# Attention, mixture of experts and mixer on one core: gate logits summed head by head inside attention instead of in a stage of their own

## The reference, cut to what matters

```python
# B=2, H=8, S=768, head width 64; 8 global keys, 96 local keys
a = softmax(scores + bias);  attn_out = a @ v                     # (B, H, S, 64)
x = attn_out.transpose(0, 2, 1, 3).reshape(B, S, H * 64)          # (2, 768, 512)
logits = einsum('bsd,de->bse', x, w_gate)                         # 8 experts
local_gate = sigmoid(einsum('bsd,de->bse', x, w_local))           # 1 more column
# e = argmax(logits) where local_gate < 0.5 or s == 0, else the expert of token s - 1
out[b, s] = softmax(logits)[e] * (relu(x[b, s] @ w1[e]) @ w2[e])
# then the mixer: theta, cos/sin, two token matmuls, a channel matmul
```

## Time and profile before

| what | value |
|---|---|
| median of three runs | 590.67 us (590.6 to 592.94) |
| the profiled execution | 590.95 us, of which 589.3 us are the span from the first to the last instruction |
| attention, up to the last `x_tok` | 0 to 111.3 us |
| logits stage | 111.3 to 135.3 us |
| routing | 135.3 to 147.8 us |
| scatter, and the first tile's way in | 147.8 to 169.5 us |
| experts and mixer | 169.5 to 589.3 us |
| busy share of the span | PE 87%, DVE 47%, ACT 34%, POOL 20% |

### The profile page before, as it was taken

How to read it: one execution, slowest core, us unless ns; L and a number is a source line. 1 busy time by engine, 2 the same in 40 slices (tenths; PEclk the granted TensorE clock), 3 DMA queues, 4 the chain that set the end, 5 groups by cost and what they waited for, 6 DMA issues and landing times.

```text
span 589.3 us, 9126 instructions
## 1 busy us (share of the span) xinstructions
PE 509.8 (87%) x3252; PEld 421.7 (72%) x3253; DVE 277.4 (47%) x606; ACT 202.2 (34%) x420; POOL 116.7 (20%) x116
## 2 busy tenths in 40 slices
PE   0899999693059999999989989937999999999987
PEld 0677777531059989899979979925788878888866
DVE  5566767315141141414253351226897877555143
ACT  1579888220201131313241331143444333222010
POOL 4967873100710020202120200045000000000000
PEclk9999999797569999999999999976999999999999
DMA  7744648640442164729297361125000000000002
GB/s 259 232 135 143 220 137 311 250 169 2 178 146 103 36 245 184 311 98 379 74 402 320 138 271 36 36 82 151 0 2 0 2 0 1 18 19 18 37 36 91
DMA packets 22563, 77.61 MB, mean 132 GB/s; under 512 B 3456, under 2 KB 3712, under 8 KB 18432
## 3 DMA queue, kind: packets, MB, share of 16 engines
q0 software_dynamic: 8032, 46.67, 20.2%
q1 hardware_dynamic: 11904, 26.31, 13.5%
q10 hardware_dynamic: 2592, 4.20, 2.1%
HBM read 61.43 MB, written 15.73 MB: 131 GB/s over the span
## 4 chain that ended last, share of the span: by engine, by line
PE 65%; issue 15%; DVE 10%; DMA 4%; ACT 3%; POOL 2%; DVEq 1%; POOLq 0%; ACTq 0%
PE ps L1163 35%; PE ps L1188 10%; PE ps L1007 5%; PE ps L1062 5%; PE ps L1046 4%; DMA w_sb<-in_w_experts 2%; PE ps L1124 2%; POOL slots L481 2%; PE ps L1027 1%; PE ps L1116 1%; PE ps L1249 1%; DVE w_lo L886 1%; PE ps L1174 1%; DMA x_tok<-slots,slot 1%; DVE z L909 1%
## 5 line engine op out<-in xcount | busy, mean ns | idle before, releaser
L1188 PEld LDWEIGHTS ps<-xT,w_sb 128*128 128x128 f32 x1024 | 118.3, 194 | 5.8 <-issue 3.3
L1188 PE MATMUL ps<-xT,w_sb 128*128 128x128 f32 x1024 | 118.9, 278 | 3.6 <-DMA w_sb<-in_w_experts 2.6
L877 DVE SCALAR_TENSOR_TENSOR hT_lo<-ps,hT_hi 128x512 fp32r<-128x512 f32 x32 | 21.8, 688 | 98.7 <-ACT hT_hi L585 98.4
L886 DVE TENSOR_TENSOR w_lo<-w_sb,w_hi 128x1024 fp32r<-128x1024 f32 x32 | 37.0, 1219 | 47.3 <-ACT w_hi L598 47.3
L1163 PE MATMUL ps<-w_hi,hT_hi 128*128 128x512 f32 x128 | 51.4, 401 | 2.2 <-DVE hT_lo L877 2.2
L532 ACT ACTIVATE prob<-raw,row_min 128x256 f32<-128x256 f32 (+1 forms) x96 | 46.2, 485 | 12.3 <-DVE row_min L745 11.3
L1163 PE MATMUL ps<-w_hi,hT_lo 128*128 128x512 f32 x128 | 50.0, 391 | 0.0
L1163 PE MATMUL ps<-w_lo,hT_hi 128*128 128x512 f32 x128 | 49.9, 390 | 0.0
L471 POOL DMA_DIRECT2D w_sb<-in_w_experts x32 | 17.3, 543 | 161.5 <-PE ps L1163 141.6
L585 ACT ACTIVATE hT_hi<-ps 128x512 fp32r<-128x512 f32 x32 | 19.1, 596 | 85.1 <-PE ps L1188 85.1
L589 ACT COPY yout<-ps 128x512 f32<-128x512 f32 x16 | 9.4, 586 | 89.8 <-PE ps L1163 89.8
(11 more groups left out here) (184 smaller groups left out, 987.9 us busy)
## 6 DMA issues: line engine op xcount, KB each, us to landing
w_sb<-in_w_experts POOLq DMA_DIRECT2D x32, 1024.0 KB, 9.7
v_sb<-in_vx SPq DMA_DIRECT2D x8, 640.0 KB, 5.0
slots<-zero SPq DMA_DIRECT2D x20, 256.0 KB, 5.2
xin<-slots SPq DMA_DIRECT2D x17, 256.0 KB, 2.7
slots<-yout ACTq DMA_DIRECT2D x16, 256.0 KB, 2.7
k_raw<-in_kx SPq DMA_DIRECT2D x8, 432.0 KB, 5.9
q_raw<-in_q SPq DMA_DIRECT2D x8, 384.0 KB, 6.3
out_x<-o_sb SPq DMA_DIRECT2D x12, 256.0 KB, 2.0
```

The source lines that it names most:

```text
L877: dve.scalar_tensor_tensor(hT_lo[:, part, :], ps[:, 1 + half, :].rearrange("p (c q) -> p c q", c=4), 0.0, hT_hi[:, part, :].bitcast(F32), ...
L886: dve.tensor_tensor(quarter(w_lo, par, q), quarter(w_sb, par, q), w2_hi_quarter(q).bitcast(F32), ALU.subtract).then_inc(s_w2_lo, 1)
L1188: last = pe.matmul(ps[:, 1 + half, f * P:(f + 1) * P], w_sb[:, par, c // 2, j:j + P], xT[:, c, :], start=(c == 0), stop=(c == DC - 1))
```

## The change

The gate weights are laid out anew on the host: for each head a block of 128 rows (64 for batch 0, 64 for batch 1) by 18 columns, with the nine gate columns of that head at rows 0 to 63, columns 0 to 8, and again at rows 64 to 127, columns 9 to 17, the rest zero. `turn_back` now follows its three transposes with three matmuls: stationary is the same block of `outT` (128 by 128), moving is the head's 18 columns, and the result lands beside the transposes in bank 7. `normalise` multiplies these 54 columns by the reciprocal denominators into `part`, ahead of `x_tok`. A new function, `add_logits`, adds `part` to `lg`: one step later than `normalise` inside the loop, directly after it at the end. The logits stage is gone with its semaphores and tiles; routing waits on VectorE's own last addition.

```diff
+SHARE = B * (E + 1)
+TURNED = GROUP * P
-        wg = sb("wg", [P, DC, E + 1])
+        wg = sb("wg", [P, H, B * (E + 1)])
+        part = sb("part", [P, 2, GROUP * B * (E + 1)])
+        lg = sb("lg", [P, NT, E + 1])
...
-            for n in range(1, NT, 2):
-                act.wait_ge(s_xt_t, n + 1)
-                act.copy(xTall[:, :, n * P:(n + 1) * P],
-                         ps[:, n % 4, :].rearrange("p (c q) -> p c q", c=DC)).then_inc(s_xt_odd, 1)
-                if n % 4 == 3:
-                    act.wait_ge(s_lgt, n // 4 + 1)
-                    act.copy(lgT[:, n // 4, :], ps[0:E + 1, 4 + n // 4, :]).then_inc(s_lgt_out, 1)
...
                 dve.wait_ge(s_back, q + 1)
                 dve.wait_ge(s_den, q + 1)
+                share = rec[:, half, :].rearrange("p (i b o) -> p i b o", i=GROUP, o=1)
+                dve.tensor_tensor(part[:, half, :].rearrange("p (i b e) -> p i b e", i=GROUP, b=B),
+                                  ps[:, 7, TURNED:TURNED + GROUP * SHARE].rearrange("p (i b e) -> p i b e", i=GROUP, b=B),
+                                  share.to_broadcast([P, GROUP, B, E + 1]), ALU.mult)
                 dve.tensor_tensor(x_tok.rearrange("p (b i) d -> p i b d", b=B)[:, tiles, :, h * DH:(h + 1) * DH],
...
+            def add_logits(q):
+                h, half = q // 2, q % 2
+                to = lg.rearrange("p (b i) e -> p i b e", b=B)[:, GROUP * half:GROUP * half + GROUP]
+                of = part[:, half, :].rearrange("p (i b e) -> p i b e", i=GROUP, b=B)
+                dve.wait_ge(s_x_done, q + 1)
+                if h == 0:
+                    dve.tensor_copy(to, of).then_inc(s_sum, 1)
+                else:
+                    dve.wait_ge(s_sum, q - 1)
+                    dve.tensor_tensor(to, to, of, ALU.add).then_inc(s_sum, 1)
...
                     if g >= 6 and g % GROUP == 0:
                         normalise(g // GROUP - 2)
+                    if g >= 6 and g % GROUP == 1:
+                        add_logits(g // GROUP - 2)
                 normalise(PAIRS // GROUP - 2)
                 second_half(PAIRS // GROUP - 1)
+                add_logits(PAIRS // GROUP - 2)
                 normalise(PAIRS // GROUP - 1)
+                add_logits(PAIRS // GROUP - 1)
...
-            dve.wait_ge(s_logits, 1)
-            then(dve.tensor_copy(lg[:], ps[:, 7, 0:NT * (E + 1)].rearrange("p (n e) -> p n e", n=NT)))
+            dve.wait_ge(s_sum, PAIRS // GROUP)
...
                 for j in range(GROUP):
-                    last = pe.transpose(ps[:, 7, j * P:(j + 1) * P], outT[:, q % 2, j * P:(j + 1) * P], ident)
+                    pe.transpose(ps[:, 7, j * P:(j + 1) * P], outT[:, q % 2, j * P:(j + 1) * P], ident)
+                if q == 0:
+                    pe.wait_ge(s_wg_in, 16)
+                for j in range(GROUP):
+                    last = pe.matmul(ps[:, 7, TURNED + j * SHARE:TURNED + (j + 1) * SHARE],
+                                     outT[:, q % 2, j * P:(j + 1) * P], wg[:, q // 2, :], start=True, stop=True)
                 last.then_inc(s_back, 1)
...
-            for n in range(NT):
-                turn_tokens(n)
-                if n in (4, 8):
-                    logits(n // 4 - 1)
-            turn_logits(0)
-            logits(2)
-            turn_logits(1)
-            turn_logits(2).then_inc(s_logits, 1)
             pe.wait_ge(s_p_ready, 1)
...
+    gates = np.concatenate([moe_w_gate, moe_w_local], axis=1).reshape(H, DH, E + 1)
+    wgx = np.zeros((B, DH, H, B, E + 1), gates.dtype)
+    for b in range(B):
+        wgx[b, :, :, b] = gates.transpose(1, 0, 2)
+    wgx = wgx.reshape(P, H * B * (E + 1))
```

More of the change, by code:

```diff
@@ L177, in program @@
         s_x_done = sem("x_done")
-        s_xt_t = sem("xt_t")
-        s_xt_even = sem("xt_even")
-        s_xt_odd = sem("xt_odd")
-        s_logits = sem("logits")
-        s_lgt = sem("lgt")
-        s_lgt_out = sem("lgt_out")
+        s_sum = sem("sum")
         s_g_act = sem("g_act")
@@ L722, in normalise @@
                 dve.wait_ge(s_den, q + 1)
+                share = rec[:, half, :].rearrange("p (i b o) -> p i b o", i=GROUP, o=1)
+                dve.tensor_tensor(part[:, half, :].rearrange("p (i b e) -> p i b e", i=GROUP, b=B),
+                                  ps[:, 7, TURNED:TURNED + GROUP * SHARE].rearrange("p (i b e) -> p i b e", i=GROUP, b=B),
+                                  share.to_broadcast([P, GROUP, B, E + 1]), ALU.mult)
                 dve.tensor_tensor(x_tok.rearrange("p (b i) d -> p i b d", b=B)[:, tiles, :, h * DH:(h + 1) * DH],
                                   ps[:, 7, 0:GROUP * P].rearrange("p (i b d) -> p i b d", i=GROUP, b=B),
-                                  rec[:, half, :].rearrange("p (i b o) -> p i b o", i=GROUP, o=1).to_broadcast([P, GROUP, B, DH]),
-                                  ALU.mult).then_inc(s_x_done, 1)
+                                  share.to_broadcast([P, GROUP, B, DH]), ALU.mult).then_inc(s_x_done, 1)
+            def add_logits(q):
[8 more added lines that the diff above has]
+                    dve.tensor_tensor(to, to, of, ALU.add).then_inc(s_sum, 1)
             def windows():
@@ L786, in whole_rows @@
                         normalise(g // GROUP)
+                        add_logits(g // GROUP)
             either(dve, windows, whole_rows)
-            for n in range(0, NT, 2):
-                dve.wait_ge(s_xt_t, n + 1)
-                dve.tensor_copy(xTall[:, :, n * P:(n + 1) * P],
-                                ps[:, n % 4, :].rearrange("p (c q) -> p c q", c=DC)).then_inc(s_xt_even, 1)
-            dve.wait_ge(s_logits, 1)
-            then(dve.tensor_copy(lg[:], ps[:, 7, 0:NT * (E + 1)].rearrange("p (n e) -> p n e", n=NT)))
+            dve.wait_ge(s_sum, PAIRS // GROUP)
             top, best, fresh, val = (gate_m[:, j, :] for j in range(4))
@@ L1107, in _ @@
             either(pe, windows, whole_rows)
-            pe.wait_ge(s_x_done, PAIRS // GROUP)
-            pe.wait_ge(s_wg_in, 16)
-            def turn_tokens(n):
-                wait(pe, (s_xt_even, s_xt_odd)[n % 2], (n - 2) // 2)
-                for c in range(DC):
-                    last = pe.transpose(ps[:, n % 4, c * P:(c + 1) * P], x_tok[:, n, c * P:(c + 1) * P], ident)
-                last.then_inc(s_xt_t, 1)
-            def logits(g):
-                pe.wait_ge(s_xt_even, 2 * (g + 1))
-                pe.wait_ge(s_xt_odd, 2 * (g + 1))
-                for c in range(DC):
-                    last = pe.matmul(ps[0:E + 1, 4 + g, :], wg[:, c, :], xTall[:, c, g * 4 * P:(g + 1) * 4 * P],
-                                     start=(c == 0), stop=(c == DC - 1))
-                last.then_inc(s_lgt, 1)
-            def turn_logits(g):
-                pe.wait_ge(s_lgt_out, g + 1)
-                for n in range(4 * g, 4 * g + 4):
-                    last = pe.transpose(ps[:, 7, n * (E + 1):(n + 1) * (E + 1)], lgT[:, g, (n % 4) * P:(n % 4 + 1) * P],
-                                        ident[0:E + 1, 0:E + 1])
-                return last
-            for n in range(NT):
-                turn_tokens(n)
-                if n in (4, 8):
-                    logits(n // 4 - 1)
-            turn_logits(0)
-            logits(2)
-            turn_logits(1)
-            turn_logits(2).then_inc(s_logits, 1)
             pe.wait_ge(s_p_ready, 1)
```

9 lines of the change are left out of this document (3 added, 6 removed).

## The result

The changed kernel takes 579.33 us (median of 4 runs, 577.81 to 583.93), the kernel before in the same measurement 590.63 us (4 runs, 589.54 to 592.94). The ratio estimated over all the runs is 0.985, 95% interval 0.9806 to 0.9895 (the two medians alone give 0.981). The forecast was 580.7 us, 575.0 to 585.5. The profiled execution takes 579.05 us with a span of 577.0, so the spans differ by 12.3 us.

What follows compares the result with a forecast made beforehand. The prediction took TensorE to bound the kernel, with the logits stage on its path. Terms -23.97 + 11.2 + 2.5 + 0.3 = -10.0 us, from the median 590.67, gave 580.7 us, range 575.0 to 585.5.

Steps and rivals of the forecast that it cites:

- The stage is on the path, and its removal comes off the end: Logits stage between attention and routing: TensorE busy 19.7 of 24.0 us, no overlap with its neighbours, so removal shortens the whole.
- Its size: Stretch from the last `x_tok` to routing's first reduction, all counted as the removed logits stage: -23.97 us.
- A pass at 0.11 us: New gate matmuls on TensorE in attention: load-paced passes of 0.11 us, six per group 0.66 us, 14 groups 9.2 us.
- Rival (a): New gate matmuls go at the faster pace of L1131's loads: 4.8 us less, 573.5 to 577.5 us; chance 0.14.
- VectorE in the tail: Last two groups of attention: `part`, matmuls and the last addition lie on the path, 1.97 us together.
- An addition that waits for GpSimd: First group's `add_logits` in a head waits 1.3 us for GpSimd, stalling TensorE up to 1.0 us; 2.5 us taken.
- The second group's addition is free: In each attention head, the second group's `add_logits` comes after GpSimd's L454 and costs nothing.
- Routing 0.3 us slower at the lower clock: Routing behind attention: TensorE idles ahead of it, so its tiny matmuls run at the lower clock, 0.3 us more.
- The stretches behind stay to within 1 us: Stretches behind routing, including scatter and experts, stay as long as before to within 1 us.
- (b): In attention VectorE or ScalarE binds more often than counted, 1.0 us in six or more heads: 584 to 588; chance 0.12.
- (d): Each first group's addition meets the start of GpSimd's L459, 3.6 us long, so the kernel is slower: 596 us; chance 0.04.
- (c): Gain partly given back behind: scatter queues behind the second expert's weights, or first tile waits: 584 to 588; chance 0.04.

Runs made afterwards that it cites:

- The routing experiment: Changed kernel with VectorE's and TensorE's routing written inside both branches of attention: 575.34 us, ratio 0.9766 to the kernel before.
- doubling: Changed kernel with the three gate matmuls of each group issued twice, 96 passes more: 588.44 us (one run).
- old kind: The kernel before, its unchanged repeat (589.12 us), and the kernel before with the changed kernel's gate load in the old one's place (588.48 us).
- filler: Changed kernel with matmuls whose result nobody reads on TensorE while tokens are scattered, in two lengths: 578.78 and 575.43 us; also tried with other edits, 573.48 us.
- new kind: The changed kernel, its unchanged repeat and the variants edited from it, against the kernel before; the unchanged kernel took 579.33 us, repeated 578.87 us.
- The repeat: Both kernels timed again without edits: changed kernel 578.87 us against 588.76 us, ratio 0.982.
- filler that ended 3.4 us short: Changed kernel with 25 useless matmuls on TensorE behind the slots: 578.78 us, ratio 0.9808 to the kernel before.
- filler up to the first real instruction: Changed kernel with 27 useless matmuls behind the slots and two behind the first tile's transposes: 575.43 us, ratio 0.977 to the kernel before.

## Why the prediction was right, point by point

- **The stage is on the path, and its removal comes off the end:** right. **Its size**, -23.97 us, was the term most off: it is -20.95. The prediction called all of the stretch between the earlier trace rows the removed stage. 2.89 us of it were not the stage's but TensorE leaving the branch, and they came back as 3.02 us on VectorE. The routing experiment takes them away. The chain of waits of the kernel before shows the piece in plain sight.
- **A pass at 0.11 us:** right as a pace, 0.112 between loads in the changed kernel, and 0.11 for each pass added by doubling. What the sum had too high is six full passes a group, 0.66 us: in its place a group costs 0.585, because about one step is absorbed at its edges. The 14 groups cost 8.2 us, not 9.2. Rival (a), the pace of L1131's loads, is wrong. That 18 and 128 streamed columns go at one pace fits with the load setting it, as the prediction argued; no run changes the number of columns loaded.
- **VectorE in the tail:** 1.6 us (last `x_tok` but two to the last addition 8.86 us, 7.28 before), not 1.97.
- **An addition that waits for GpSimd:** the alignment was right, and in every head; the length was wrong. The step that failed is "such VectorE operations wait out the GpSimd operation in flight": beside L463 the addition waits 0.47 us, not 1.3, and that reaches TensorE as 0.1 us a head, not 1.0. The rows it was read from could not tell: L698 was beside a GpSimd TENSOR_TENSOR, L459, and L467 (L463 now) is a TENSOR_SCALAR. The term is 0.5 to 0.6 us instead of 2.5. The prediction's sign of being wrong about the wait ("no addition is longer than 0.3 us") did not appear, and still the size was off by more than a factor of four.
- **The second group's addition is free:** in time, yes; but it does wait for q_lo, and `den_e` for q_hi.
- **Routing 0.3 us slower at the lower clock:** 0.2. **Routing starts near 125 us:** it was 121.4, the sum of the misses above and of the start.
- **The stretches behind stay to within 1 us:** to 0.2 us from the slots on, and the scatter was not held up by the second weights; but the first tile took 1.1 us more. By the letter the sign "if the time from the slots to the first w1 pass grows" appeared, by 0.2 us. The prediction did not look at how TensorE comes back to the higher clock. Most of that 1.1 us need not be the change's: without a filler the first w1 set took 9.12 to 9.17 us in the three profiles of the old kind, and 10.2 (three times), 9.93, 9.72, 9.01, 8.96 and 8.87 in those of the new kind, whose programs do not differ there. In the changed kernel the granted clock is 0.52 in 160 to 162 us and 1.00 in 162 to 164, inside the set. What sets that moment stays open.
- **The median:** the terms as measured give -20.95 + 8.2 + 1.6 + 0.55 + 0.2 + 0.2 + 1.1 + 0.1 = -9.0 us without the start, whose 3.3 us were for the most part one execution's luck. The repeat has -9.9 us, the first measurement -11.3. The forecast of -10.0 is right by misses of both signs: 3 us too much removed, 1.4 too much added, 1.95 too much waited, 1.1 missed in the first tile.

Rivals (b) and (d) had a true mechanism, VectorE's lead does get used up (ScalarE waits for it ten times, has one), but its excess over TensorE stays at tenths. (c) did not occur in the scatter, and by 1.1 us in the first tile.

## What to carry to other kernels

Before a stage's whole stretch is booked as a gain, look in the chain of waits for pieces of "issue" in it: those that belong to the control flow around the stage stay when the stage goes, and only move to the next engine. Here writing the code that follows into the branch was worth a third of the whole change, 3.5 us beside 9.9. When an elementwise operation with two SBUF inputs is slipped in beside GpSimd's, work out its moment, but price the wait by what reaches the bounding engine, and not by how long the operation itself is held. When passes are added in a row, their pace is not yet their price: look at what the row's two ends cost. And where TensorE idles ahead of a dense stage, filler has to reach it: here filler that ended 3.4 us short gave nothing, and filler up to the first real instruction took 2.8 us off the first set.

## What the runs showed of the hardware that was not expected

- Leaving an If/Else branch costs an engine about 3 us with nothing else to wait for: 2.89, 2.53 and 2.48 us on TensorE in the three profiles of the old kind, 2.66 to 3.23 on VectorE in eight of the new.
- In the first 23 to 36 us, over fourteen profiles, matmuls go at half pace (a batch of 8 in 1.12 us, later 0.66) although the profile gives the granted clock as 1.00 there; the moment of the change differed by 5 us between two executions of one kernel.
- A GpSimd TENSOR_TENSOR holds up a VectorE operation with two SBUF inputs to its end, even one of 6 columns (0.15 us becomes 1.10). A TENSOR_SCALAR of 1.50 us held one that began with it for 0.47 us, and one that began 0.69 us after it not at all (0.21 us).
- Real fp32 passes with 128 columns loaded start 0.112 us apart with 18 columns streamed as with 128, and 0.12 us apart with 146. A group of them costs less or more than its passes by what its ends cost: 0.58 us for six behind the transposes, 0.94 for six of 146 columns at a group's start.
